# Router logits of 15 token tiles: from TensorE (turns and 8-column matmuls) to VectorE (multiply-and-sum) in a fused attention, MLP and expert kernel

## The chip, the cores and the metric

One core of a Trainium2 chip runs the whole kernel as one program. The metric is the device time of one execution in microseconds (us); lower is better.

## The reference, cut to what matters

Three layers follow each other: a sparse attention, a gated MLP on the normed rows, and a top-1 mixture of experts whose router reads the MLP's output rows. What the change touches is the line with `logits`.

```python
x = attention(q, k, v)                                  # 2304 tokens x 512
x = silu(rmsnorm(x) @ w_gate) * (rmsnorm(x) @ w_val) @ w_out   # inner width 1536
logits = x @ router_w + router_bias[modality_id]        # router_w: 512 x 8
e_idx = argmax(logits, axis=1)
gate_w = softmax(logits)[row, e_idx]
out[row] = gate_w * (relu(x @ w1[e_idx]) @ w2[e_idx])
```

All products are in fp32 precision: a large operand is split into a high and a low part (`_hi`, `_lo`) and three matmuls take the place of one.

## The kernel before, in words

**Chunks, tiles and steps.** The MLP takes the 2304 tokens in NC = 6 chunks (0 to 5) of 384 tokens; a chunk is TT = 3 tiles of 128 tokens. In each chunk it goes over the inner width in FT = 12 steps f of 128 columns. The order of the work is written out by hand, for each engine in its own queue, by a clock of half steps: a step has 6 of them (`at(c, f, sub, half)`), a chunk 72. Engines don't share a clock; the numbers only set the order of instructions in each queue, and semaphores do the rest. In one step TensorE (PE) makes the gate product (12 matmuls, half steps 0 and 1, L1100), the value product (12 matmuls, half steps 2 and 3, L1100) and the down product of the step before (9 matmuls, half steps 4 and 5, L1139); the last step of a chunk has two down products.

**The loop between engines.** ScalarE takes tanh of the gate product (L1276). VectorE multiplies it into the gate (`scale_gate`, L1418, half step 2), forms h with the value product (`form_h`, L1424, half step 4), ScalarE rounds h to its high part (L1280), and VectorE takes the low part (`h_split`, L1429, half step 5). PE's gate product of step f + 1 waits for `scale_gate` of f, its value product of f + 1 for `form_h` of f, and the down product of f for `h_split` of f. GpSimd (POOL) splits each block of `w_out` into `out_hi` (L936) and `out_lo` (L938) once a step. SyncE (SP) issues the loads and the stores of the y tiles to the scratch rows x2.

**Other work.** The attention of later batches is spread over the steps of chunks 0 to 3. At each chunk's end VectorE finds the norms of the next chunk (`roots` L1384 to L1395, `normalise_x` L1405, `x_split` L1412); POOL squares its rows (L918 to L925).

**The router's logits before.** The y of chunk c (ys, 3 tiles) is evacuated by ScalarE at the start of chunk c + 1 (L1288). During chunk c + 1 each of its tiles is turned by PE with 4 transposes (`turn_y`, L1150), evacuated by ScalarE (L1293), multiplied by the router's weights in 4 matmuls of 8 columns (`logits`, L1159; each leaves two records), and VectorE adds the bias (`add_bias`, L1437). So 15 tiles (those of chunks 0 to 4) pass through PE; the 3 tiles of chunk 5 are done after the MLP, and stay as they are. These turns and products share PSUM bank 7 with the attention and the norms.

**What follows.** In step 3 of chunk 5 (HOT_1, its half step 23 counted from 0) VectorE starts the early routing on the 15 tiles (`one_hot`, L595 to L605); PE counts it (L652, L653) at the start of the value product of step 4. The experts' loop follows the MLP.

Of the kernel before, what the change touches and what calls it, by code (L numbers as in the profile page):

```python
# [13 lines left out]
KT = DM // P  # L14
# [9 lines left out]
G = B * NG  # L24
SM = 4
# [30 lines left out]
def at(c, f, sub, half=0):  # L56
    return EARLY + SPAN * c + 6 * f + 2 * sub + half
# [29 lines left out]
def qk_ticks(b, hp):  # L87
# [3 lines left out]
    if s < EARLY:  # L91
# [20 lines left out]

SS = {0: 16, **{c + 1: at(c, 9, 2) for c in range(NC - 1)}}
SPREAD = {c: s + (2 if c == 0 else 6) for c, s in SS.items()}
Y_TILE = {(c, t): at(c + 1, 3 + 2 * t, 2) if c < NC - 2 else at(c + 1, 1 + t, 0)
          for c in range(NC - 1) for t in range(TT)}
LOGITS = {k: s + 2 for k, s in Y_TILE.items()}
SS_AT = by_tick((c, s) for c, s in SS.items())
SPREAD_AT = by_tick((c, s) for c, s in SPREAD.items())
Y_AT = by_tick((k, s) for k, s in Y_TILE.items())  # L120
LOGITS_AT = by_tick((k, s) for k, s in LOGITS.items())
BANK7 = [x for s in range(TICKS) for x in
         [("p", j) for j in TURN_AT.get(s, [])] + [("o", j) for j in PV_AT.get(s, []) if s >= EARLY]
         + [("ss", c) for c in SS_AT.get(s, []) if c] + [("rb", c) for c in SPREAD_AT.get(s, []) if c]
         + [("y", k) for k in Y_AT.get(s, [])] + [("lg", k) for k in LOGITS_AT.get(s, [])]]
# [27 lines left out]
def fused_kernel(nc, q, k, v, w_gate, w_val, w_out, rms_g, modality_id, router_w, router_bias, w1, w2, x2, out):  # L153
# [4 lines left out]
    with ctx:  # L158
# [61 lines left out]
        hh = [res.put(f"h_hi{i}", [P, CH], f32r) for i in range(2)]  # L220
        hl = [alias(f"h_lo{i}", hf_at + i * CH * 4, [P, CH], f32r) for i in range(2)]
        yT_at = res.at
        yT = res.put("yT", [P, KT, P])
        sq_at = res.at
        sq = res.put("sq", [P, CH])
        diag = alias("diagonals", sq_at, [P, TT, P])
# [15 lines left out]
        vstr = [res.put(f"vstr{i}", [SQ, 2, SU * D]) for i in range(2)]  # L242
        qT = [res.put(f"qT{i}", [P, S]) for i in range(2)]
        kT = [res.put(f"kT{i}", [P, WIN + S]) for i in range(2)]
        sm = [res.put(f"sm{i}", [P, 512]) for i in range(SM - 1)] + [alias("sm_early", yT_at, [P, 512])]
        pt = [res.put(f"pt{i}", [P, 4 * LQ]) for i in range(2)]
        mask_loc = res.put("mask_loc", [LQ, 2, P])
        mask_str = res.put("mask_str", [SQ, SQ])
# [160 lines left out]
        s_ye = sem("y_evacuated")  # L409
        s_x2 = sem("y_stored")  # L410
        s_bu = sem("bias_built")
        s_yt = sem("y_tile_turned")
        s_yte = sem("yT_evacuated")
        s_lg = sem("logits_of_tile")
        s_le = sem("logits_read")

        SQS = 2 * KT - 2
# [332 lines left out]
        def front_sp(sp):  # L750
# [91 lines left out]
            for s in range(TICKS):  # L842
                for b, hp in QK_LOAD_AT.get(s, []):
                    qk_loads(b, hp)
                for b, hp in V_LOAD_AT.get(s, []):
                    v_loads(b, hp)
                if s >= EARLY:
                    c, f, sub, half = step_of(s)
                    if (sub, half) == (0, 0) and FT * c + f + 1 < FT * NC:
                        out_load(FT * c + f + 1)  # L850
                    if c and (f, sub, half) == (0, 2, 0):
                        store(c - 1)
                if s == W_LOAD_1:
                    early_weights(sp)
            store(NC - 1)
# [107 lines left out]
        def front_pe(pe):  # L963

            def bank_7_free(what):

                before = BEFORE7[what]
                if before is None:
                    return
                if before[0] == "p":  # L970
                    pe.wait_ge(s_pe, before[1] + 1)
                elif before[0] == "o":
                    pe.wait_ge(s_oe, before[1] + 1)
                elif before[0] == "ss":
                    pe.wait_ge(s_nv, before[1] + 1)
                elif before[0] == "rb":
                    pe.wait_ge(s_xn, KT * before[1] + KT)
                elif before[0] == "y":
                    pe.wait_ge(s_yte, TT * before[1][0] + before[1][1] + 1)
                else:  # L980
                    pe.wait_ge(s_le, TT * before[1][0] + before[1][1] + 1)

            def residues():
                pe.wait_ge(s_ms, 2)
# [156 lines left out]
                if ts[-1] == TT - 1:  # L1141
                    mm.then_inc(s_y, 1)

            def turn_y(c, t):

                if t == 0:
                    pe.wait_ge(s_ye, c + 1)
                bank_7_free(("y", (c, t)))
                for kk in range(KT):
                    mm = pe.transpose(ps[:, 7, kk * P:(kk + 1) * P], ys[:, t, kk * P:(kk + 1) * P], ident[:, :])  # L1150
                mm.then_inc(s_yt, 1)

            def logits(c, t):
                bank_7_free(("lg", (c, t)))
                if c == 0 and t == 0:
                    pe.wait_ge(s_small, 48)
                pe.wait_ge(s_yte, TT * c + t + 1)
                for kk in range(KT):
# [15 lines left out]
            for s in range(TICKS):  # L1174
                if s < EARLY:
                    for key in QK_AT.get(s, []):
                        turn_qk(*key)
                for j in SCORE_AT.get(s, []):
                    score(j)
                for j in TURN_AT.get(s, []):  # L1180
                    turn_probs(j)
                for j in PV_AT.get(s, []):
                    values(j)
                if s >= EARLY:
                    for key in QK_AT.get(s, []):
# [7 lines left out]
                for key in Y_AT.get(s, []):
                    turn_y(*key)
                for key in LOGITS_AT.get(s, []):
                    logits(*key)
# [33 lines left out]
        def front_act(act):  # L1230
# [51 lines left out]
            def evac_y(c):  # L1282

                act.wait_ge(s_y, FT * c + FT)
                if c:
                    act.wait_ge(s_x2, 16 * TT * c)
                    act.wait_ge(s_yt, TT * c)
                act.activation(ys[:, :, :], ps[:, 2:2 + TT, :], ACT.Copy).then_inc(s_ye, 1)  # L1288

            def evac_yT(c, t):  # L1290

                act.wait_ge(s_yt, TT * c + t + 1)
                act.activation(yT[:, :, :].rearrange("p k n -> p (k n)"), ps[:, 7, :],  # L1293
                               ACT.Copy).then_inc(s_yte, 1)

            for s in range(TICKS):
                c, f, sub, half = step_of(s) if s >= EARLY else (0, 0, -1, 0)
# [8 lines left out]
                if s >= EARLY:  # L1306
                    for key in QK_AT.get(s, []):
                        dst, src = evac_qk(act, *key)
                        act.activation(dst, src, ACT.Copy).then_inc(s_qe, 1)
                for key in Y_AT.get(s, []):  # L1310
                    evac_yT(*key)
                if s == SPREAD[0] + 1:
                    x_split(0)
                for j in EXPS_AT.get(s, []):
# [13 lines left out]
        def front_dve(dve):  # L1328
# [100 lines left out]
                dve.tensor_tensor(hl[n % 2][:, :], hf[n % 2][:, :], hh[n % 2][:, :].bitcast(f32),  # L1429
                                  ALU.subtract).then_inc(s_hl, 1)  # L1430

            def add_bias(c, t):
                i = TT * c + t
                if i == 0:
                    dve.wait_ge(s_bu, 6)
                dve.wait_ge(s_lg, i + 1)
                dve.tensor_tensor(logit[:, i, :], ps[:, 7, 0:E], bias_t[:, i, :], ALU.add).then_inc(s_le, 1)  # L1437

            for s in range(TICKS):
                c, f, sub, half = step_of(s) if s >= EARLY else (0, 0, -1, 0)  # L1440
# [485 lines left out]
```

## Time and profile before

| | us |
|---|---|
| median of 3 runs | 930.52 (927.36 to 930.64) |
| the profiled execution, its time | 929.51 |
| its span | 927.7 |
| PE busy | 898.6 (97%) |
| DVE busy | 456.4 (49%) |
| ACT busy | 360.9 (39%) |
| POOL busy | 308.1 (33%) |

A row of instructions gives line, engine, operation, the tile written and the tiles read, their shapes and the count; behind the bar it has the busy time in us, the mean of one in ns and the idle time of the engine before them. A row of the timeline gives start, duration, and, in square brackets, the idle time before it with what released it. PEld is the load of TensorE's weights; PEclk is the granted clock of TensorE as a share of full speed.

### The profile page before, as it was taken

How to read it: one execution, taken by the hardware profiler on the slowest of the kernel's cores; microseconds unless marked ns; L12 is line 12 of the kernel's file. 1: busy time of each engine (PE TensorE's matmuls, PEld its weight loads, DVE VectorE, ACT ScalarE, POOL GpSimd, SP SyncE). 2: the span in 40 equal slices, each digit the busy share in tenths (PEclk: the TensorE clock that was granted, in tenths of full speed). 3: DMA queues.
4: the chain of work that ended last, by engine and by line, in shares of the span. 5: the costliest groups of instructions: out<-in, count | busy, mean ns of one | idle time of the engine just before them, and what ended most of it. 6: DMA issues, size and time to landing. Idle time of an engine off the chain costs nothing.

```text
span 927.7 us, 15901 instructions
## 1 busy us (share of the span) xinstructions
PE 898.6 (97%) x5433; PEld 767.6 (83%) x5433; DVE 456.4 (49%) x1239; ACT 360.9 (39%) x935; POOL 308.1 (33%) x366
## 2 busy tenths in 40 slices
PE   8989999999999999999999999999789999999996
PEld 5657898888878888799999999998678888888884
DVE  5864555433454345522433343774754466446651
ACT  5866413544444444421121131242243355335430
POOL 2734762344233342344234233240502222212221
PEclk9999999999999999999999999999889999999998
DMA  8972212222113211211121121610836355515521
GB/s 180 276 188 77 58 51 65 66 65 73 49 44 107 61 27 32 67 36 36 35 80 35 39 75 35 222 51 35 302 135 242 129 182 189 201 48 197 194 74 35
DMA packets 74486, 94.95 MB, mean 102 GB/s; under 512 B 38701, under 2 KB 42797, under 8 KB 74416
## 3 DMA queue, kind: packets, MB, share of 16 engines
q1 hardware_dynamic: 70656, 82.51, 29.2%
q0 software_dynamic: 3760, 11.54, 3.6%
q8 instruction: 40, 0.66, 0.3%
q14 instruction: 30, 0.25, 0.1%
HBM read 84.59 MB, written 10.22 MB: 102 GB/s over the span
## 4 chain that ended last, share of the span: by engine, by line
PE 90%; DVE 4%; ACT 1%; issue 1%; POOL 1%; DMA 1%; ACTq 0%; POOLq 0%; DVEq 0%
PE ps L1100 34%; PE ps L1139 15%; PE ps L1575 13%; PE ps L1590 11%; PE ps L1032 3%; PE ps L1061 2%; PE ps L1602 2%; PE ps L1042 2%; PE ps L1009 2%; PE ps L1166 1%; PE ps L1159 1%; PE ps L569 1%; PE ps L1150 1%; DMA xg<-x_rows,idx_gather 1%; DVE h_lo L1429 0%
## 5 line engine op out<-in xcount | busy, mean ns | idle before, releaser
L1418 DVE SCALAR_TENSOR_TENSOR h<-h,ps 128x384 f32<-128x384 f32 x72 | 39.9, 554 | 175.2 <-ACT h L1276 175.1
L906 POOL TENSOR_TENSOR sm<-sm,rinv 72x288 f32<-72x288 f32 (+1 forms) x51 | 45.6, 894 | 204.2 <-DVE rinv L1362 204.1
L1100 PE MATMUL ps<-x_hi,gate_hi 128*128 128x384 f32 x288 | 104.1, 362 | 0.0
L1100 PE MATMUL ps<-x_hi,val_hi 128*128 128x384 f32 x288 | 102.1, 354 | 0.0
L936 POOL CAST out_hi<-out_raw 128x512 fp32r<-128x512 f32 x72 | 46.6, 648 | 155.1 <-DMA out_raw<-in_moe_w_out 155.1
L1100 PE MATMUL ps<-x_hi,gate_lo 128*128 128x384 f32 x288 | 97.5, 338 | 0.0
L938 POOL TENSOR_TENSOR out_lo<-out_raw,out_hi 128x512 fp32r<-128x512 f32 x72 | 95.1, 1322 | 5.8
L1100 PE MATMUL ps<-x_hi,val_lo 128*128 128x384 f32 x288 | 96.9, 337 | 0.0
L1100 PE MATMUL ps<-x_lo,val_hi 128*128 128x384 f32 x288 | 96.9, 336 | 0.0
L1100 PE MATMUL ps<-x_lo,gate_hi 128*128 128x384 f32 x288 | 94.4, 338 | 0.0
L1139 PE MATMUL ps<-out_hi,h_hi 128*128 128x512 f32 x216 | 89.4, 414 | 2.1 <-DVE h_lo L1429 2.1
L1429 DVE TENSOR_TENSOR h_lo<-h,h_hi 128x384 fp32r<-128x384 f32 x72 | 64.4, 895 | 43.5 <-ACT h_hi L1280 43.5
L1139 PE MATMUL ps<-out_hi,h_lo 128*128 128x512 f32 x216 | 85.3, 395 | 0.0
L1139 PE MATMUL ps<-out_lo,h_hi 128*128 128x512 f32 x216 | 84.9, 393 | 0.0
L1532 POOL DMA_INDIRECT out_rows<-yo,idx_s x21 | 21.7, 1032 | 179.0 <-DVE yo L1766 177.2
L1280 ACT ACTIVATE h_hi<-h 128x384 fp32r<-128x384 f32 x72 | 37.7, 524 | 105.6 <-DVE h L1424 105.6
L1261 ACT ACTIVATE sm<-sm,nmin 72x72 f32<-72x72 f32 (+1 forms) x204 | 73.3, 363 | 12.1 <-DVE nmin L1351 12.0
L1424 DVE SCALAR_TENSOR_TENSOR h<-h,ps 128x384 f32<-128x384 f32 x72 | 39.9, 554 | 68.5 <-PE ps L1100 68.3
L1276 ACT ACTIVATE h<-ps 128x384 f32<-128x384 f32 x72 | 34.9, 484 | 98.6 <-PE ps L1100 98.4
L1739 DVE TENSOR_TENSOR w_lo<-w_raw,w_hi 128x1024 fp32r<-128x1024 f32 x60 | 69.4, 1220 | 4.2 <-ACT w_hi L1666 4.0
L1590 PE MATMUL ps<-w_hi,hT_hi 128*128 128x512 f32 x168 | 68.1, 405 | 0.0
L1590 PE MATMUL ps<-w_lo,hT_hi 128*128 128x512 f32 x168 | 66.4, 395 | 0.0
(248 smaller groups left out, 1926.2 us busy)
## 6 DMA issues: line engine op xcount, KB each, us to landing
w_raw<-in_moe_w SPq DMA_DIRECT2D x64, 512.0 KB, 6.6
out_raw<-in_moe_w_out SPq DMA_DIRECT2D x72, 256.0 KB, 2.6
x_rows<-y_tiles SPq DMA_DIRECT2D x18, 256.0 KB, 2.4
early_w_raw<-in_moe_w SPq DMA_DIRECT2D x8, 512.0 KB, 6.1
gate_raw<-in_moe_w_gate SPq DMA_DIRECT2D x4, 768.0 KB, 9.8
val_raw<-in_moe_w_val SPq DMA_DIRECT2D x4, 768.0 KB, 9.5
qk<-in_q SPq DMA_DIRECT2D x8, 288.0 KB
qk<-in_k SPq DMA_DIRECT2D x8, 288.0 KB
```

The costliest lines, as they stand in the source:

```text
L906: pool.tensor_tensor(s3, s3, rinv[0:n, i, :].unsqueeze(2).to_broadcast([n, 4, c]), ALU.mult).then_inc(s_no, 1)
L936: pool.tensor_copy(oh[i][:, :], o_raw[i][:, :]).then_inc(s_oh, 1)
L938: pool.tensor_tensor(ol[i][:, :], o_raw[i][:, :], oh[i][:, :].bitcast(f32), ALU.subtract).then_inc(s_ol, 1)
L1100: mm = pe.matmul(ps[:, bank, 0:CH], w[:, i, kk, cols], x[:, kk, :], start=(m == 0), stop=(m == n - 1))
L1139: mm = pe.matmul(ps[:, 2 + t, :], a[:, cols], w[:, :], start=(f == 0 and i == 0), stop=(f == FT - 1 and i == 2))
L1261: act.activation(s2, s2, ACT.Exp, scale=-1.0, bias=nmin[0:n, k_, i:i + 1], accum_out=rsum[0:n, k_, i:i + 1]).then_inc(s_ex, 1)
L1418: dve.scalar_tensor_tensor(out=hf[n % 2][:, :], in0=hf[n % 2][:, :], scalar=1.0, in1=ps[:, 0, 0:CH], op0=ALU.add, op1=ALU.mult).then_inc(s ...
L1424: dve.scalar_tensor_tensor(out=hf[n % 2][:, :], in0=hf[n % 2][:, :], scalar=0.5, in1=ps[:, 1, 0:CH], op0=ALU.mult, op1=ALU.mult).then_inc( ...
L1429: dve.tensor_tensor(hl[n % 2][:, :], hf[n % 2][:, :], hh[n % 2][:, :].bitcast(f32), ALU.subtract).then_inc(s_hl, 1)
L1575: mm = pe.matmul(ps[:, half, :], x[:, kk, :], w[:, kk, half * 512:(half + 1) * 512], start=(kk == 0 and n == 0), stop=(kk == KT - 1 and n ...
L1590: mm = pe.matmul(ps[:, 5, :], x[:, j, :], w[:, j, :], start=(j == 0 and n == 0), stop=(j == FJ - 1 and n == 2))
L1739: dve.tensor_tensor(lo[:, i * n:(i + 1) * n, :], raw[:, i * n:(i + 1) * n, :], hi[:, i * n:(i + 1) * n, :].bitcast(f32), ALU.subtract).the ...
```

## The change

The 15 tiles leave PE. For each tile and each of the 8 experts, VectorE multiplies the tile (128 tokens by 512) by the expert's router column, spread over all partitions, and sums along the row: 120 instructions of 512 elements, with the product written to a tile that nobody reads. The column is taken from `rw_all` [128, 512, 8] with a step of 8 elements (32 bytes). `rw_all` is loaded once, 16 KB for each of 128 partitions. Tiles 0 to 8 (chunks 0 to 2) are loaded back from the scratch rows into three buffers; tiles 9 to 14 are read where they lie. The dot products of tiles 0 to 11 stand at one per half step from step 5 of chunk 3 to step 8 of chunk 4, those of tiles 12 to 14 at three in two half steps from half step 4 to 19 of chunk 5. Each waits for the one before it. ScalarE's evacuation of y waits for the logits in chunk 5 only; PE's waits on bank 7 for turns and logits go. `sm_early` gets a place of its own in the room of `yT`.

```diff
-Y_TILE = {(c, t): at(c + 1, 3 + 2 * t, 2) if c < NC - 2 else at(c + 1, 1 + t, 0)
-          for c in range(NC - 1) for t in range(TT)}
-LOGITS = {k: s + 2 for k, s in Y_TILE.items()}
...
+RELOADED = TT * (NC - 3)
+ROUTER = at(NC - 3, 4, 0)
+DOT = {(i, e): at(NC - 3, 5, 0) + E * i + e if i < TT * (NC - 2)
+       else at(NC - 1, 0, 2) + (E * (i - TT * (NC - 2)) + e) * 2 // 3
+       for i in range(TT * (NC - 1)) for e in range(E)}
+DOT_AT = by_tick((k, s) for k, s in DOT.items())
+DOTTED_AT = by_tick((i, DOT[i, E - 1] + 1) for i in range(TT * (NC - 1)))
+RELOAD_AT = by_tick((i, DOT[i, 0] - 8) for i in range(RELOADED))
...
+                if s == ROUTER:
+                    sp.wait_ge(s_oe, G)
+                    sp.dma_start(rw_all[:, :, :].rearrange("p d e -> p (d e)"),
+                                 router_w.rearrange("d e -> (d e)").partition_broadcast(P)).then_inc(s_rwa, 16)
+                for i in RELOAD_AT.get(s, []):
+                    if i >= 3:
+                        sp.wait_ge(s_le, i - 2)
+                    sp.wait_ge(s_x2, 16 * TT * (i // TT + 1))
+                    sp.dma_start(y_again[i % 3][:, :], x2[i * P:(i + 1) * P, :]).then_inc(s_ya[i % 3], 16)
...
-            def turn_y(c, t):
...
-                    mm = pe.transpose(ps[:, 7, kk * P:(kk + 1) * P], ys[:, t, kk * P:(kk + 1) * P], ident[:, :])
...
-                    mm = pe.matmul(ps[:, 7, 0:E], yT[:, kk, :], rw[:, kk, :],
-                                   start=(kk == 0), stop=(kk == KT - 1))
...
-                    act.wait_ge(s_yt, TT * c)
+                if c > NC - 3:
+                    act.wait_ge(s_le, TT * c)
...
+            def dot(i, e):
+
+                if e == 0 and i < RELOADED:
+                    dve.wait_ge(s_ya[i % 3], 16 * (i // 3) + 16)
+                if e == 0 and i >= RELOADED:
+                    dve.wait_ge(s_ye, i // TT + 1)
+                if (i, e) == (0, 0):
+                    dve.wait_ge(s_rwa, 16)
+                if E * i + e:
+                    dve.wait_ge(s_dot, E * i + e)
+                if e == 0 and i >= 2:
+                    dve.wait_ge(s_le, i - 1)
+                y = y_again[i % 3][:, :] if i < RELOADED else ys[:, i % TT, :]
+                dve.tensor_tensor_reduce(out=unread[:, :], in0=y, in1=rw_all[:, :, e], scale=1.0, scalar=0.0,
+                                         op0=ALU.mult, op1=ALU.add,
+                                         accum_out=dots[:, i % 2, e:e + 1]).then_inc(s_dot, 1)
...
-                dve.tensor_tensor(logit[:, i, :], ps[:, 7, 0:E], bias_t[:, i, :], ALU.add).then_inc(s_le, 1)
+                dve.wait_ge(s_dot, E * i + E)
+                dve.tensor_tensor(logit[:, i, :], dots[:, i % 2, :], bias_t[:, i, :], ALU.add).then_inc(s_le, 1)
```

## Rows read from the trace of the kernel before

**Rows 1.** The page: busy time, and the chain that ended last.
```profile
PE 898.6 (97%) x5433; PEld 767.6 (83%) x5433; DVE 456.4 (49%) x1239; ACT 360.9 (39%) x935; POOL 308.1 (33%) x366
...
PE 90%; DVE 4%; ACT 1%; issue 1%; POOL 1%; DMA 1%; ACTq 0%; POOLq 0%; DVEq 0%
```
**Rows 2.** Windows: stretch, its length, busy us, PEclk, DMA share, GB/s.
```profile
415.43:524.40 108.97, 108.97 (x603) 102.15 (x603) 35.18 (x74) 21.81 (x42) 38.19 (x41) 1.00 0.16 46
...
559.32:566.90 7.58, 7.58 (x48) 7.14 (x47) 1.75 (x4) 1.62 (x3) 3.73 (x12) 1.00 0.12 35
...
580.77:587.04 6.27, 6.27 (x35) 5.88 (x34) 5.55 (x22) 0.49 (x1) 1.94 (x2) 1.00 0.45 145
```
**Rows 3.** Chain in order of time, chunks 3 to 5: start, us, what.
```profile
409.05 4.30 PE ps L1100 x24
...
524.43 4.18 PE ps L1100 x24
...
574.29 2.11 PE ps L1100 x12
```
**Rows 4.** Groups of VectorE by shape, whole span.
```profile
L1351 DVE CUSTOM_DVE_ANT_0 sm<-ps,mask_loc 96x128 f32<-96x128 f32 x92 | 21.1, 282 | 6.8 <-PE ps L1032 6.6
L1351 DVE CUSTOM_DVE_ANT_0 sm<-ps,mask_str 72x72 f32<-72x72 f32 x112 | 19.1, 224 | 9.1 <-PE ps L1032 9.1
L682 DVE TENSOR_TENSOR sel<-in_tile,star 128x120 f32<-128x120 f32 x1 | 0.4, 357 | 0.0
L690 DVE TENSOR_TENSOR sel<-hot,star 128x120 f32<-128x120 f32 x1 | 0.3, 283 | 0.0
L1793 DVE TENSOR_TENSOR before<-upto,in_tile 128x144 f32<-128x144 f32 x1 | 0.3, 309 | 0.0
L1794 DVE TENSOR_TENSOR rank<-before,ps 128x144 f32<-128x144 f32 x1 | 0.4, 416 | 0.0
```
**Rows 5.** Timeline of VectorE: two instructions linked by a semaphore.
```profile
449.88 0.16 DVE L1391 TENSOR_TENSOR newton<-newton,variance 128x3 f32<-128x3 f32 x1
450.08 0.16 DVE L1392 SCALAR_TENSOR_TENSOR root<-newton,root 128x3 f32<-128x3 f32 x1
```
**Rows 6.** Timeline of VectorE and POOL at 391 and 399 us.
```profile
391.50 0.78 DVE L1429 TENSOR_TENSOR h_lo<-h,h_hi 128x384 fp32r<-128x384 f32 x1 [0.59 <-ACT h_hi L1280]
...
399.65 1.67 DVE L1429 TENSOR_TENSOR h_lo<-h,h_hi 128x384 fp32r<-128x384 f32 x1 [0.59 <-ACT h_hi L1280]
...
391.26 0.61 POOL L936 CAST out_hi<-out_raw 128x512 fp32r<-128x512 f32 x1
...
399.62 1.29 POOL L938 TENSOR_TENSOR out_lo<-out_raw,out_hi 128x512 fp32r<-128x512 f32 x1
```
**Rows 7.** POOL by shape, 415.43 to 524.40 us.
```profile
L938 POOL TENSOR_TENSOR out_lo<-out_raw,out_hi 128x512 fp32r<-128x512 f32 x16 | 20.6, 1288 | 1.3
L936 POOL CAST out_hi<-out_raw 128x512 fp32r<-128x512 f32 x16 | 9.8, 614 | 67.4 <-DMA out_raw<-in_moe_w_out 67.4
```
**Rows 8.** Timeline of VectorE in chunk 5.
```profile
551.66 0.55 DVE L1424 SCALAR_TENSOR_TENSOR h<-h,ps 128x384 f32<-128x384 f32 x1 [1.07 <-PE ps L1100]
...
569.79 0.55 DVE L1418 SCALAR_TENSOR_TENSOR h<-h,ps 128x384 f32<-128x384 f32 x1 [3.36 <-ACT h L1276]
...
573.46 0.56 DVE L1429 TENSOR_TENSOR h_lo<-h,h_hi 128x384 fp32r<-128x384 f32 x1 [0.59 <-ACT h_hi L1280]
573.93 0.27 DVE L595 TENSOR_REDUCE top<-bias_then_logit 128x15 f32<-128x120 f32 x1
...
575.87 0.22 DVE L605 CAST hot_b<-hot 128x120 bf16<-128x120 f32 x1
```
**Rows 9.** Loads: KB each, median us to landing; and GB/s in 40 slices.
```profile
x_rows<-y_tiles SPq DMA_DIRECT2D x18, 256.0 KB, 2.4
...
GB/s 180 276 188 77 58 51 65 66 65 73 49 44 107 61 27 32 67 36 36 35 80 35 39 75 35 222 51 35 302 135 242 129 182 189 201 48 197 194 74 35
```
**Rows 10.** Window of the experts' first slots, columns as in group 2.
```profile
667.00:690.00 23.00, 19.49 (x69) 15.40 (x70) 13.26 (x14) 10.76 (x13) 4.97 (x8) 0.73 0.40 145
```

More of the change, by code:

```diff
@@ L114 @@
 SPREAD = {c: s + (2 if c == 0 else 6) for c, s in SS.items()}
-Y_TILE = {(c, t): at(c + 1, 3 + 2 * t, 2) if c < NC - 2 else at(c + 1, 1 + t, 0)
-          for c in range(NC - 1) for t in range(TT)}
-LOGITS = {k: s + 2 for k, s in Y_TILE.items()}
 SS_AT = by_tick((c, s) for c, s in SS.items())
 SPREAD_AT = by_tick((c, s) for c, s in SPREAD.items())
-Y_AT = by_tick((k, s) for k, s in Y_TILE.items())
-LOGITS_AT = by_tick((k, s) for k, s in LOGITS.items())
 BANK7 = [x for s in range(TICKS) for x in
          [("p", j) for j in TURN_AT.get(s, [])] + [("o", j) for j in PV_AT.get(s, []) if s >= EARLY]
-         + [("ss", c) for c in SS_AT.get(s, []) if c] + [("rb", c) for c in SPREAD_AT.get(s, []) if c]
-         + [("y", k) for k in Y_AT.get(s, [])] + [("lg", k) for k in LOGITS_AT.get(s, [])]]
+         + [("ss", c) for c in SS_AT.get(s, []) if c] + [("rb", c) for c in SPREAD_AT.get(s, []) if c]]
 BEFORE7 = {x: BANK7[n - 1] if n else None for n, x in enumerate(BANK7)}
@@ L222, in fused_kernel @@
         yT_at = res.at
-        yT = res.put("yT", [P, KT, P])
+        sm_early = res.put("sm_early", [P, 512])
         sq_at = res.at
@@ L244, in fused_kernel @@
         kT = [res.put(f"kT{i}", [P, WIN + S]) for i in range(2)]
-        sm = [res.put(f"sm{i}", [P, 512]) for i in range(SM - 1)] + [alias("sm_early", yT_at, [P, 512])]
+        sm = [res.put(f"sm{i}", [P, 512]) for i in range(SM - 1)] + [sm_early]
         pt = [res.put(f"pt{i}", [P, 4 * LQ]) for i in range(2)]
@@ L309, in fused_kernel @@
         at_pos_1 = alias("at_pos_1", vl_at, [P, EARLY_TILES, P], f32r)
+        ra = Region(xT_at + KT * 2 * S * 4)
+        rw_all = ra.put("router_on_all", [P, DM, E])
+        y_again = [ra.put(f"y_again{i}", [P, DM]) for i in range(3)]
+        unread = ra.put("unread", [P, DM])
+        dots = ra.put("dots", [P, 2, E])
         re = Region(xT_at)
@@ L411, in fused_kernel @@
         s_bu = sem("bias_built")
-        s_yt = sem("y_tile_turned")
-        s_yte = sem("yT_evacuated")
-        s_lg = sem("logits_of_tile")
+        s_rwa = sem("router_on_all_loaded")
+        s_ya = [sem(f"y_loaded_again{i}") for i in range(3)]
+        s_dot = sem("dot_products")
         s_le = sem("logits_read")
@@ L975, in bank_7_free @@
                     pe.wait_ge(s_nv, before[1] + 1)
-                elif before[0] == "rb":
+                else:
                     pe.wait_ge(s_xn, KT * before[1] + KT)
[L978 to L981, printed above, removed]
             def residues():
@@ L1142, in down @@
                     mm.then_inc(s_y, 1)
-            def turn_y(c, t):
[L1146 to L1149, printed above, removed]
-                    mm = pe.transpose(ps[:, 7, kk * P:(kk + 1) * P], ys[:, t, kk * P:(kk + 1) * P], ident[:, :])
[L1151 to L1158, printed above, removed]
-                    mm = pe.matmul(ps[:, 7, 0:E], yT[:, kk, :], rw[:, kk, :],
-                                   start=(kk == 0), stop=(kk == KT - 1))
-                mm.then_inc(s_lg, 1)
             def keep_busy(n):
@@ L1192, in front_pe @@
                     spread_roots(c)
[L1193 to L1196, printed above, removed]
                 if s == COUNT_1:
@@ L1286, in evac_y @@
                     act.wait_ge(s_x2, 16 * TT * c)
-                    act.wait_ge(s_yt, TT * c)
+                if c > NC - 3:
+                    act.wait_ge(s_le, TT * c)
                 act.activation(ys[:, :, :], ps[:, 2:2 + TT, :], ACT.Copy).then_inc(s_ye, 1)
[L1290 to L1294, printed above, removed]
             for s in range(TICKS):
@@ L1309, in front_act @@
                         act.activation(dst, src, ACT.Copy).then_inc(s_qe, 1)
-                for key in Y_AT.get(s, []):
-                    evac_yT(*key)
                 if s == SPREAD[0] + 1:
@@ L1430, in h_split, with add_bias @@
                                   ALU.subtract).then_inc(s_hl, 1)
-            def add_bias(c, t):
-                i = TT * c + t
+            def dot(i, e):
[13 more added lines that the diff above has]
+                                         accum_out=dots[:, i % 2, e:e + 1]).then_inc(s_dot, 1)
+            def add_bias(i):
                 if i == 0:
                     dve.wait_ge(s_bu, 6)
-                dve.wait_ge(s_lg, i + 1)
-                dve.tensor_tensor(logit[:, i, :], ps[:, 7, 0:E], bias_t[:, i, :], ALU.add).then_inc(s_le, 1)
+                dve.wait_ge(s_dot, E * i + E)
+                dve.tensor_tensor(logit[:, i, :], dots[:, i % 2, :], bias_t[:, i, :], ALU.add).then_inc(s_le, 1)
             for s in range(TICKS):
@@ L1460, in front_dve @@
                     invert(j)
-                for key in LOGITS_AT.get(s, []):
-                    add_bias(*key)
+                for key in DOT_AT.get(s, []):
+                    dot(*key)
+                for i in DOTTED_AT.get(s, []):
+                    add_bias(i)
                 for val, i in SPLIT_AT.get(s - 2, []):
```

## The prediction

> **What bounds the kernel now.** I read the page first: PE is busy 97% of the span, and 90% of the chain that ended last is PE [rows 1]. So work taken from PE is worth its full time, as long as no other engine takes its place. Then the windows of single steps: a plain step of the MLP takes 6.27 us, and a step of chunk 5 that also has one tile's turns and logits takes 7.58 [rows 2]. In order of time the chain of chunks 3 to 5 is PE throughout, product behind product [rows 3]. So the difference of 1.31 us lies on the path. VectorE is the other engine to watch: in the 16 steps that will hold most of the new work (step 5 of chunk 3 to step 8 of chunk 4, 415.43 to 524.40 us) it is busy 35.2 of 109.0 us, and POOL 38.2 [rows 2].
>
> **What is removed.** One tile costs PE 7.58 - 6.27 = 1.31 us, so 15 tiles are 19.7 us. By place: 7 tiles lie before the new work (chunk 1, chunk 2, the first one in chunk 3), 5 in the 16 steps, 3 in chunk 5. Only the first 7 are surely on the path afterwards: -9.2 us. ScalarE's 15 evacuations and VectorE's waits for the logits go too, at nothing: PE hid them.
>
> **What one dot product costs.** The same operation stands in the attention (L1351): 282 ns for 128 elements and 224 for 72 [rows 4]. That is 58 ns for 56 elements, 1.04 ns each, and 149 ns fixed; 512 contiguous elements are 0.68 us. But the router column is read with a step of 8 elements, and no row has that. The nearest rows are two pairs of small instructions of one size of which one reads an SBUF tile with a step: L682 (step 15) takes 357 ns and L690 283 for 120 elements, L1794 (step 18) 416 and L1793 309 for 144 [rows 4]. The extra is 0.62 and 0.74 ns per element. Bounds: nothing, if a step of 32 bytes on the second input is free, to 0.74 and perhaps more; I take 0.68, since both pairs agree: 0.35 us for 512. Each dot product waits for its predecessor by semaphore; linked instructions start 0.20 us apart at 0.16 each [rows 5], so 0.04 us is added. Sum: 0.68 + 0.35 + 0.04 = 1.07 us (0.72 without the step's extra).
> The Trainium skill, "Vector Engine (DVE) Microarchitecture Reference", section on measured stream behaviour (the access granule), says that a port keeps its rate only on pairs of adjacent words, gives 1.73 ns per column for one source hopping at every element, and 2.50 for steps of 24 words on both sources. By 1.73 a dot product would again be some 1.07 us, by 2.50 it would be 1.47 and the time below some 48 us longer (estimates from that page); no row here has steps in this form of instruction.
>
> **What POOL adds.** The dot product reads both inputs from SBUF, as L1429 does. L1429 takes 0.56 us alone [rows 8], but 1.67 when it starts 0.03 us after POOL's L938 (1.29 us), and it then ends 0.41 us behind it; started 0.24 us into L936 (0.61 us) it takes 0.78 [rows 6]. So VectorE waits until POOL is through, for about POOL's time less 0.15: 1.14 and 0.46, 1.6 us per step. The 9 other POOL instructions of the 16 steps are the squares: 38.2 - 20.6 - 9.8 = 7.8 us [rows 2, 7], 6.4 after the same cut. Together 16 x 1.6 + 6.4 = 32 us. About a seventh of VectorE's time is in operations with an input in PSUM that don't wait; I take 27 us (bounds: 0, if the dot product doesn't share what L1429 shares, and 32).
> The Trainium skill, "SBUF — State Buffer", who interferes with whom, has the second to issue block for the whole instruction, which would make it 1.9 us per step and some 4 us more in all (an estimate); the rows show 0.15 less per instruction.
>
> **The 16 steps.** VectorE's work: 35.2 us that it has, 7 more biases at 0.2 = 1.4, 96 dot products x 1.07 = 102.7, POOL 27: 166 us, against 109 that PE takes now and 102 without its 5 tiles. VectorE becomes the bound: some 10.4 us per step. It can't fall behind for free, since PE's gate product of the next step waits for `scale_gate`, which is queued behind the dot products, as are `form_h` and `h_split`. Start: the first dot product waits for `rw_all`. SP issues it when down(2) of chunk 3 ends, just before 409.05 less the logits, 408.3 [rows 3]. Its 2.1 MB at the highest rate of a slice, 302 GB/s, are 6.9 us, and 1.5 fixed (a 256 KB transfer takes 2.4) [rows 9]: it lands at 416.7, 1.5 us after VectorE wants it, hidden in part by the 4 us that PE leaves `scale_gate` (569.79 against the gate product at 574.29) [rows 3, 8]. 416.7 + 166.3 = 583.0. PE's gate product of step 9 needs only `scale_gate` of step 8, ahead of the last 4 dot products, `form_h`, `h_split`, a bias and some POOL: -6.6; then its value product waits 0.8 for `form_h`. PE is there at 577.2 where it was at 524.4 [rows 3]: +52.8 us. The 9 reloads of 256 KB take 2.4 us each [rows 9] and are asked for 8 half steps ahead: nothing, and SP's wait for `logits_read` ahead of them is met by then. Steps 9 to 11 hold no dot products; VectorE recovers and they stay as they are.
>
> **Chunk 5.** 24 dot products follow `form_h` of step 0 (ends at 552.2 [rows 8]) and must be done before `scale_gate` of step 3: 24 x 1.07 = 25.7, the MLP's own 5.0 (h_split, two steps of 1.67, `scale_gate`, three biases), POOL 3 x 1.6 less a seventh = 4.1. `scale_gate` ends at 587.0, and the gate product of step 4, at 574.29 now [rows 3], starts then: +12.8. The one-hot (573.93 to 576.1 [rows 8]) comes behind `h_split` of step 3, at 589.3, and ends at 591.3; PE is through the gate product at 589.2 and waits 2.1. Together +14.9.
>
> **Sum.** The profiled execution took 929.51, 1.0 less than the median and inside the runs shown: 929.5 - 9.2 + 52.8 + 14.9 = 988 us.
>
> **The rivals.**
> *The step is dear, POOL's turns cost nothing* (for: other ports than L1429's; against: same two inputs in SBUF). VectorE's 16 steps are 139.3 us instead of 166.3: +26.8 (the tail is 1 us shorter too). Chunk 5 without its 4.1: 8.7 + 2.1 = +10.8. 958 us.
> *The step is free, POOL costs* (for: no row with a step of 8 or on the second input; against: two pairs of rows). 96 x 0.72 = 69.1: sum 132.7, +20.1 with the shorter tail. Chunk 5: 24 x 0.72 = 17.3, so `scale_gate` ends at 578.6, 4.3 + 2.1 = +6.4. 947 us.
> *VectorE keeps up: faster.* One mechanism: reads at the full rate, and no waiting on POOL. Then 35.2 + 1.4 + 69.1 = 105.7 us of VectorE stand against 102.4 of PE, the 16 steps end 6.2 us earlier than now, chunk 5 is +0.2 (552.2 + 17.3 + 5.0 = 574.5) and the 2.1 at the count: 929.5 - 9.2 - 6.2 + 2.3 = 916 us. It is decided by the price of one dot product with its share of POOL: the 16 steps break even at (109.0 - 36.6) / 96 = 0.75 us; the rows say 1.07 + 0.28.
> *The step costs twice what the pairs show* (1.36 ns): a dot product of 1.42 us; 16 steps 52.8 + 96 x 0.35, less 1.4 in the tail, +85; chunk 5 14.9 + 24 x 0.35 = +23: 1029 us.
> *PE loses its clock.* With PE at work 6.3 of 10.4 us a step, its granted clock could fall, as to 0.73 in a stretch where it was busy 19.5 of 23 us with its idle time in long pieces [rows 10]. At 1.2 GHz a step is 12.5 us of PE, more than VectorE's 10.4: 16 steps +92, 1027 us. Against it: the gaps here are some 1 to 2 us each.
>
> **How the numbers follow.** Forecast (step dear, POOL in the way) 0.62; POOL free 0.10; step free 0.10; keeps up 0.07; step twice as dear 0.06; clock 0.05. 0.5% is about what a measurement of this kernel can tell from no change. Faster holds only where VectorE keeps up: 0.06, and 0.02 for a case between it and the others that lands within 0.5%; slower 0.92. The forecast's own spread is 975 to 1003 (0.62 to 0.74 per element, POOL 20 to 32 us). The range goes down to 945 (step free) and up to 1030 (twice as dear, clock); keeps up and what lies past 1030 are left out.
>
> **What the profile after would show.** Right: a dot product of about 1.03 us as shown, 1.35 to 1.4 a piece with POOL's share; steps of 10 us in chunks 3 and 4 with PE waiting for `scale_gate`, `form_h` and `h_lo`; VectorE without idle time there; POOL's L936 and L938 longer, since they wait too; the steps of chunk 2 without L1150 and L1159, 1.3 us shorter for each tile. Wrong: dot products of 0.68 us; VectorE idle in the 16 steps; a first dot product that starts long after 417 (the load of `rw_all` slow); PEclk under 1.00 in chunk 4; a wait for y tiles loaded again.

## The result, and the profile after

The changed kernel takes 987.05 us (median of 4 runs, 986.77 to 990.26) against 928.94 before (4 runs, 925.44 to 930.64): a ratio of 1.063, 95% interval 1.0594 to 1.0667. It is slower, 1 us from the forecast of 988.

The page of the changed kernel, to be held against [rows 1]: TensorE fell from 97% to 91%, VectorE rose by 149 us.

```profile
span 985.0 us, 15777 instructions
...
PE 900.8 (91%) x5253; PEld 754.4 (77%) x5253; DVE 605.5 (61%) x1479; ACT 351.5 (36%) x920; POOL 340.4 (35%) x366
```

Windows of the changed kernel; the columns are those of [rows 2]. The second is the 16 steps (from the tanh of step 5 of chunk 3 to that of step 9 of chunk 4), the third chunk 5 up to the tanh of step 5.

```profile
169.39:411.12 241.73, 237.64 (x1611) 202.81 (x1610) 104.09 (x392) 106.46 (x361) 92.19 (x100) 1.00 0.23 68
411.12:570.63 159.51, 117.30 (x544) 98.20 (x543) 154.92 (x268) 17.72 (x37) 66.02 (x43) 0.95 0.14 45
593.47:643.93 50.46, 36.22 (x160) 31.69 (x159) 43.49 (x89) 5.05 (x11) 13.45 (x19) 0.86 0.13 42
```

The same stretches of the kernel before:

```profile
166.46:417.57 251.11, 247.06 (x1695) 211.98 (x1694) 107.47 (x398) 109.80 (x368) 91.08 (x100) 1.00 0.20 56
417.57:526.58 109.01, 109.01 (x604) 102.19 (x603) 35.18 (x74) 21.82 (x43) 38.19 (x41) 1.00 0.16 46
549.50:582.92 33.42, 33.42 (x196) 31.57 (x195) 13.58 (x39) 7.08 (x15) 9.85 (x19) 1.00 0.20 63
```

The reader is to see VectorE: 35.2 of 109.0 us before, 154.9 of 159.5 after. Ahead of the dot products the kernel is 9.4 us shorter, in the 16 steps 50.5 longer, in the last stretch 17.0 longer: 58.1 in all. The spans differ by 57.3; the rest is in the loads at the start and in the experts' part, see below.

Who TensorE waited for in the changed kernel from 400 to 645 us (line, what it waited for, us in total, times, the longest):

```profile
PE ps L1117 <- DVE h L1405: 29.2, 15, 3.6
PE ps L1156 <- DVE h_lo L1416: 12.8, 10, 8.6
PE ps L1117 <- DVE h L1411: 9.0, 14, 2.2
...
PE ps L664 <- DVE hot_b L617: 2.3, 1, 2.3
```

These are `scale_gate`, `h_split` and `form_h` (L1418, L1429 and L1424 before), and the one-hot that the count waits for. The longest wait (8.6 us, over at 481.27) lies at the end of chunk 3, where VectorE also makes the norms of chunk 4. One step of VectorE and POOL shows how the time is spent (timelines, start and duration):

```profile
434.20 0.54 DVE L1405 SCALAR_TENSOR_TENSOR h<-h,ps 128x384 f32<-128x384 f32 x1
434.66 1.14 DVE L1432 CUSTOM_DVE_ANT_0 unread<-y_again,router_on_all 128x512 f32<-128x512 f32 x1
...
435.84 1.15 DVE L1432 CUSTOM_DVE_ANT_0 unread<-y_again,router_on_all 128x512 f32<-128x512 f32 x1
...
436.90 0.56 DVE L1411 SCALAR_TENSOR_TENSOR h<-h,ps 128x384 f32<-128x384 f32 x1
437.37 1.18 DVE L1432 CUSTOM_DVE_ANT_0 unread<-y_again,router_on_all 128x512 f32<-128x512 f32 x1
438.46 0.10 DVE L1432 DVE_READ_ACCUMULATOR2_ANT dots<- 128x1 f32 x1
438.46 1.27 DVE L1440 TENSOR_TENSOR bias_then_logit<-dots,bias_then_logit 128x8 f32<-128x8 f32 x1
```
```profile
436.43 1.03 POOL L957 CAST out_hi<-out_raw 128x512 fp32r<-128x512 f32 x1 [8.74 <-DMA out_raw<-in_moe_w_out]
437.55 2.16 POOL L959 TENSOR_TENSOR out_lo<-out_raw,out_hi 128x512 fp32r<-128x512 f32 x1
```

The dot products take 1.14 to 1.18 us, not 1.03. POOL's out_hi stands behind a dot product and comes through while VectorE is in L1411, which reads PSUM; its out_lo (1.29 us alone) lasts 2.16, since it stands behind the next dot product, and then it is the small bias addition, 8 elements from two SBUF tiles, that waits for it: 1.27 us where the addition from PSUM took 0.17.

### The profile page after: what moved, and what is told of

Same layout as the page of the kernel before. It is cut to its first block and busy times, and to the rows that moved or that the text cites. A ratio compares the mean times of both kernels' runs of the same rounds, so it can differ in the third digit from the quotient of the medians.

```text
span 985.0 us, 15777 instructions
## 1 busy us (share of the span) xinstructions
PE 900.8 (91%) x5253; PEld 754.4 (77%) x5253; DVE 605.5 (61%) x1479; ACT 351.5 (36%) x920; POOL 340.4 (35%) x366
## 5 line engine op out<-in xcount | busy, mean ns | idle before, releaser
L1117 PE MATMUL ps<-x_hi,gate_hi 128*128 128x384 f32 x288 | 106.8, 371 | 29.2 <-DVE h L1405 29.2
L957 POOL CAST out_hi<-out_raw 128x512 fp32r<-128x512 f32 x72 | 57.5, 798 | 183.5 <-DMA out_raw<-in_moe_w_out 183.5
L1405 DVE SCALAR_TENSOR_TENSOR h<-h,ps 128x384 f32<-128x384 f32 x72 | 39.7, 552 | 122.7 <-ACT h L1270 122.7
L959 POOL TENSOR_TENSOR out_lo<-out_raw,out_hi 128x512 fp32r<-128x512 f32 x72 | 110.8, 1538 | 5.8
L1117 PE MATMUL ps<-x_hi,val_hi 128*128 128x384 f32 x288 | 104.2, 362 | 9.0 <-DVE h L1411 9.0
L1156 PE MATMUL ps<-out_hi,h_hi 128*128 128x512 f32 x216 | 90.8, 421 | 15.0 <-DVE h_lo L1416 14.9
L1432 DVE CUSTOM_DVE_ANT_0 unread<-y_again,router_on_all 128x512 f32<-128x512 f32 x72 | 90.7, 1259 | 3.0 <-DMA router_on_all<-in_moe_w_gate 1.8
L1416 DVE TENSOR_TENSOR h_lo<-h,h_hi 128x384 fp32r<-128x384 f32 x72 | 68.7, 955 | 29.2 <-ACT h_hi L1274 29.2
L1117 PEld LDWEIGHTS ps<-x_hi,gate_hi 128*128 128x128 f32 x288 | 55.9, 194 | 39.5 <-DVE h L1405 35.6
L1117 PEld LDWEIGHTS ps<-x_hi,val_hi 128*128 128x128 f32 x288 | 54.7, 190 | 17.6 <-DVE h L1411 14.1
```

Of the source, the lines that this page charges most:

```text
L957: pool.tensor_copy(oh[i][:, :], o_raw[i][:, :]).then_inc(s_oh, 1)
L959: pool.tensor_tensor(ol[i][:, :], o_raw[i][:, :], oh[i][:, :].bitcast(f32), ALU.subtract).then_inc(s_ol, 1)
L1117: mm = pe.matmul(ps[:, bank, 0:CH], w[:, i, kk, cols], x[:, kk, :], start=(m == 0), stop=(m == n - 1))
L1156: mm = pe.matmul(ps[:, 2 + t, :], a[:, cols], w[:, :], start=(f == 0 and i == 0), stop=(f == FT - 1 and i == 2))
L1405: dve.scalar_tensor_tensor(out=hf[n % 2][:, :], in0=hf[n % 2][:, :], scalar=1.0, in1=ps[:, 0, 0:CH], op0=ALU.add, op1=ALU.mult).then_inc(s ...
L1432: dve.tensor_tensor_reduce(out=unread[:, :], in0=y, in1=rw_all[:, :, e], scale=1.0, scalar=0.0, op0=ALU.mult, op1=ALU.add, accum_out=dots[ ...
```

## The experiments

One number of a whole run can mislead here: on the chip of the experiments the kernel before ran from 921.09 to 942.32 us (23 runs beside the first four; all but one under 932). In the ten profiles the first tanh of chunk 0 starts anywhere from 61.9 us (before) to 68.3, also for kernels that are the same up to there (61.9 and 67.8 in the first two below). So each profile is also read by stretches, from the starts of the 72 tanh records (L1276 before). All in us:

| kernel | chunk 1 to step 5 of chunk 3 | 16 steps | chunk 4, 9 to 11 | chunk 5, to step 4 | to step 5 |
|---|---|---|---|---|---|
| before | 251.1 | 109.0 | 22.9 | 26.9 | 6.5 |
| changed | 241.7 | 159.5 | 22.8 | 40.9 | 9.6 |
| e1_dense | 243.5 | 121.4 | 23.0 | 30.1 | 10.5 |
| e2_nosplit | 241.8 | 142.7 | 22.3 | 38.9 | 9.5 |
| e3_dense_nosplit | 243.3 | 109.2 | 23.0 | 27.6 | 11.6 |
| e4_no_dots | 241.7 | 102.3 | 23.0 | 23.0 | 6.5 |
| e5_pe_kept | 251.0 | 161.5 | 22.9 | 41.3 | 9.6 |
| e6_mix | 252.7 | 101.3 | 22.9 | 26.9 | 6.5 |
| e8_mix7 | 249.7 | 103.3 | 23.0 | 25.6 | 6.5 |

**Contiguous columns (e1_dense).**

```diff
+                        act.activation(rw_cols[:, e, :], rw_all[:, :, e], ACT.Copy).then_inc(s_rc, 1)
...
-                dve.tensor_tensor_reduce(out=unread[:, :], in0=y, in1=rw_all[:, :, e], scale=1.0, scalar=0.0,
+                dve.tensor_tensor_reduce(out=unread[:, :], in0=y, in1=rw_cols[:, e, :], scale=1.0, scalar=0.0,
```

> The changed kernel with one thing undone: ScalarE copies each router column once into a contiguous tile (8 copies), and all 120 dot products read that. Theory (the step of 32 bytes is dear): a dot product falls from 1.08 to 1.16 us to 0.68, 120 x 0.44 = 53 us less work for VectorE, which still bounds the 16 steps through its turns with POOL; 935 to 950 us. Rival (the step is free, the instruction is simply slow with two SBUF inputs): dot products stay at 1.1 us and the time at 987.

Measured: 938.88 us (2 runs), ratio to before 1.0122 (1.0054 to 1.019). By shape, dot products of this kernel:

```profile
L1438 DVE CUSTOM_DVE_ANT_0 unread<-y_again,router_columns 128x512 f32<-128x512 f32 x72 | 61.6, 855 | 6.5 <-ACT router_columns L1310 5.0
```

The mean is 0.855 us with the waits for POOL in it; undisturbed ones take 0.68 to 0.70. The step in the router tile alone is worth 38 us in the 16 steps. The kernel is still slower than before.

**POOL out of the way (e2_nosplit).** ScalarE makes out_hi of blocks 41 to 63, POOL leaves them, and TensorE takes out_hi a second time in place of out_lo.

```diff
+                if n in BY_ACT:
+                    return
...
+                    act.activation(oh[n % NW][:, :], o_raw[n % NW][:, :], ACT.Copy).then_inc(s_oa, 1)
...
-                    for i, (a, w) in enumerate(((hh[n % 2], oh[n % NW]), (hh[n % 2], ol[n % NW]),
+                    for i, (a, w) in enumerate(((hh[n % 2], oh[n % NW]), (hh[n % 2], (oh if n in BY_ACT else ol)[n % NW]),
```

> The changed kernel, columns stepped, but in the steps with dot products (block 41 to 63 of w_out) ScalarE makes out_hi, POOL does nothing with the block, and TensorE multiplies by out_hi where it took out_lo: the low part of those blocks is left out, TensorE's work is the same. Theory (POOL and VectorE exclude each other on operations with two SBUF inputs): 23 x 1.6 us less one seventh = some 30 us less; 955 to 962 us, no dot product above 1.25 us but beside the squares. Rival (POOL isn't in the way): 987 us.

Measured: 966.61 us (2 runs), ratio 1.0421 (1.0351 to 1.0491): the theory's direction, but 5 us outside its range. The 16 steps are 16.9 us shorter (159.5 to 142.7), not 27; the squares' 6.4 us at most are still in it. Groups of VectorE by shape in the 16 steps, first of the changed kernel:

```profile
L1416 DVE TENSOR_TENSOR h_lo<-h,h_hi 128x384 fp32r<-128x384 f32 x16 | 17.6, 1101 | 0.0
...
L1440 DVE TENSOR_TENSOR bias_then_logit<-dots,bias_then_logit 128x8 f32<-128x8 f32 x11 | 6.6, 598 | 0.0
```

then of this one:

```profile
L1448 DVE CUSTOM_DVE_ANT_0 unread<-y_again,router_on_all 128x512 f32<-128x512 f32 x72 | 85.3, 1185 | 2.8 <-DMA router_on_all<-in_moe_w_gate 1.6
...
L1432 DVE TENSOR_TENSOR h_lo<-h,h_hi 128x384 fp32r<-128x384 f32 x16 | 8.9, 558 | 0.0
...
L1456 DVE TENSOR_TENSOR bias_then_logit<-dots,bias_then_logit 128x8 f32<-128x8 f32 x11 | 2.4, 219 | 0.0
```

POOL had cost h_lo 8.7 us (17.6 - 8.9) and the bias additions 4.2. The 72 dot products on reloaded tiles fell from 90.7 to 85.3 us only. With POOL gone they still take 1.18 on the mean, and 1.08 to 1.23 where no square runs beside them: that is the price of the step.

**Both (e3_dense_nosplit).** The two diffs above together.

> Both edits at once: contiguous columns, and blocks 41 to 63 of w_out split by ScalarE alone (their low part is left out). Theory: VectorE's work in the 16 steps is 36.6 + 96 x 0.72 + 6 = 112 us against 102 for TensorE, so the loss is nearly gone: 915 to 925 us, faster than before. Rival (dot products delay scale_gate, form_h and h_lo by their place in the queue even where VectorE has time): above 930 us.

Measured: 924.29 us (10 runs), ratio 0.9979 (0.9946 to 1.0012): no difference from before that can be told. The 16 steps are at 109.2, as before, not at TensorE's 102.3 (e4_no_dots). TensorE's waits in this kernel, 400 to 645 us:

```profile
PE ps L1170 <- DVE h_lo L1438: 5.3, 2, 4.9
PE ps L673 <- DVE hot_b L626: 2.7, 1, 2.7
PE ps L1128 <- DVE h L1427: 2.6, 3, 1.1
```

VectorE is busy 96.0 of the 109.2 us, and TensorE waits 6.4 of them. Most of that is one wait:

```profile
460.73 1.19 PE L1170 MATMUL ps<-out_hi,h_hi 128*128 128x512 f32 x2 [4.89 <-DVE h_lo L1438]
```

It lies at the end of chunk 3, where VectorE also makes the norms of chunk 4 and POOL's squares lengthen dot products to 1.19 us. The start, with ScalarE's copies and the router's load, costs 1.1 us. So the two costs account for the loss; what is left is mostly one place where the dot products, spread evenly, meet other work of VectorE. A spacing that spares this place was not tried with all 15 tiles.

**TensorE's part alone (e4_no_dots).** No dot products, no loads for them.

```diff
-DOT_AT = by_tick((k, s) for k, s in DOT.items())
+DOT_AT = {}
...
-                dve.tensor_tensor(logit[:, i, :], dots[:, i % 2, :], bias_t[:, i, :], ALU.add).then_inc(s_le, 1)
+                dve.tensor_scalar(logit[:, i, :], bias_t[:, i, :], 1.0, None, ALU.mult).then_inc(s_le, 1)
```

> TensorE's part of the change alone: turns and logits of the 15 tiles gone, and no dot products and no loads for them; the early routing runs on the bias alone, so the experts' part does other work and only the time up to its start is read. Theory (each tile is 1.31 us on the path everywhere, attention included): the stretch from chunk 1's first tanh to that of step 5 of chunk 5 is 15 x 1.31 = 19.7 us shorter than before, and evenly so: 9.2 before step 5 of chunk 3, 6.6 in the 16 steps, 3.9 in chunk 5. Rival (in chunks 1 to 3 the attention's waits take some back): under 8 us before step 5 of chunk 3.

Measured by stretches: 9.45 us, 6.68 and 3.97, 20.1 in all from chunk 1's first tanh (1.34 a tile). The theory holds, the rival falls: the attention takes nothing back. (The run's own 956.58 us, one run, say nothing here: with the bias alone for logits the experts' part is another.)

**VectorE's part alone (e5_pe_kept).** The kernel before with the dot products and loads of the change, TensorE keeping its turns and logits.

```diff
                 for key in LOGITS_AT.get(s, []):
                     add_bias(*key)
+                for key in DOT_AT.get(s, []):
+                    dot(*key)
+                for i in DOTTED_AT.get(s, []):
+                    take_dots(i)
```

> VectorE's part alone: the kernel before with all 120 dot products, their loads and waits added, their result not used; TensorE keeps turns and logits. Theory (VectorE bounds the 16 steps, TensorE has time there): the 16 steps stay at 159 us as in the changed kernel, only the 9.3 us before them come back: 996 us. Rival (both engines' work adds up): 987 + 19.7 = 1007 us.

Measured: 993.17 us (2 runs), ratio 1.0692 (1.0629 to 1.0756), near the theory's 996 and far from the rival's 1007. The 16 steps take 161.5 us with TensorE's tiles and 159.5 without them: of the 6.6 us taken from TensorE there, 2.0 count. In chunk 5 0.4 of 3.9 count.

**The price of a step (e7_steps).** Expert e's product reads with a step of e + 1 elements, so its logits are others.

```diff
+                st = e + 1
+                col = rw_all[:, 0:DM * st // E, :].rearrange("p d e -> p (d e)").rearrange(
+                    "p (d s) -> p d s", s=st)[:, :, 0]
+                pair = (y, col) if i % 2 == 0 else (col, y)
```

> Price list: the changed kernel, but expert e's dot product reads the router tile with a step of e + 1 elements (1 to 8) instead of always 8 with its own column, as second input in even tiles and as first in odd ones; the logits are those of other numbers. Theory (any step over one element costs the same 0.4 us and more): 0.68 us at step 1, 1.08 to 1.18 at 2 to 8, first or second input alike. Rivals: the price grows with the step; or it is there on the second input alone.

The kernel took 976.46 us (one run; with other logits its experts' part is another). Two tiles on the timeline of this kernel, with the stepped tile as second input from 484.97 us (step 1) on, and as first from 496.20 on:

```profile
484.97 0.69 DVE L1436 CUSTOM_DVE_ANT_0 unread<-y_again,router_on_all 128x512 f32<-128x512 f32 x1
...
485.70 0.69 DVE L1436 CUSTOM_DVE_ANT_0 unread<-y_again,router_on_all 128x512 f32<-128x512 f32 x1
...
486.79 0.83 DVE L1436 CUSTOM_DVE_ANT_0 unread<-y_again,router_on_all 128x512 f32<-128x512 f32 x1
...
487.67 1.07 DVE L1436 CUSTOM_DVE_ANT_0 unread<-y_again,router_on_all 128x512 f32<-128x512 f32 x1
...
489.13 1.13 DVE L1436 CUSTOM_DVE_ANT_0 unread<-y_again,router_on_all 128x512 f32<-128x512 f32 x1
...
496.20 0.69 DVE L1436 CUSTOM_DVE_ANT_0 unread<-router_on_all,y_again 128x512 f32<-128x512 f32 x1
...
496.93 0.69 DVE L1436 CUSTOM_DVE_ANT_0 unread<-router_on_all,y_again 128x512 f32<-128x512 f32 x1
...
498.01 0.84 DVE L1436 CUSTOM_DVE_ANT_0 unread<-router_on_all,y_again 128x512 f32<-128x512 f32 x1
```

The theory fell in its wording: a step of 2 costs nothing (0.69, as step 1), a step of 3 costs 0.15 us, steps of 4 to 8 cost 0.4 to 0.5 (undisturbed 1.05 to 1.20), and first or second input are alike. It is no matter of "any step", but neither does it go on growing.

**A version meant to beat both (e6_mix, e8_mix7).** VectorE takes only tiles of which it has room for, from the y tiles in place, with contiguous columns; the rest stays on TensorE. The 6-tile version:

```diff
+          for c in range(NC - 1) for t in range(TT) if c not in (2, 3)}
...
+DOT = {(i, e): at(3, 5, 0, 1) + (E * (i - 6) + e) * 5 // 3 if i < 9
+       else at(4, 0, 1, 1) + (E * (i - 9) + e) * 11 // 4
+       for i in range(6, 12) for e in range(E)}
```

> A version meant to beat both: only tiles 6 to 11 (chunks 2 and 3) go to VectorE, from where they lie, with contiguous columns, 48 dot products at 5/3 and 11/4 half steps apart; the other 9 tiles stay on TensorE; nothing is loaded back. Theory (what decides is whether VectorE's step, 1.67 + 3.6 x 0.72 + 1.6 = 5.9 us at most, stays under TensorE's 6.27): 6 x 1.31 = 7.9 us less than before, 920 to 924 us. Rival (any queue of dot products ahead of scale_gate costs): 928 us or more.

Measured: 923.52 us (12 runs), ratio 0.9959 (0.9925 to 0.9993). From chunk 1 to step 5 of chunk 5 it is 6.1 us shorter than before, of 7.9. The start of the dot products held ScalarE and VectorE for some 4 us while the router's tile was under way, but TensorE waited only 0.25 us there. The wait that counts is again at the end of chunk 3:

```profile
463.17 0.47 PE L1160 MATMUL ps<-out_hi,h_hi 128*128 128x512 f32 x1 [1.44 <-DVE h_lo L1457]
```

So the next expectation puts this wait in the wrong place. The 7-tile version starts later and adds one tile:

```diff
-DOT = {(i, e): at(3, 5, 0, 1) + (E * (i - 6) + e) * 5 // 3 if i < 9
-       else at(4, 0, 1, 1) + (E * (i - 9) + e) * 11 // 4
-       for i in range(6, 12) for e in range(E)}
+DOT = {(i, e): at(3, 5, 2) + (E * (i - 6) + e) * 3 // 2 if i < 9
+       else at(4, 0, 1, 1) + (E * (i - 9) + e) * 11 // 4 if i < 12
+       else at(5, 0, 2) + 2 * e
+       for i in DOTTED for e in range(E)}
```

> The 6-tile version with two edits: its first dot product (and ScalarE's copies of the columns) 3 half steps later, since both engines waited there for the router's load and TensorE lost 1.4 us behind h_lo, and one tile of chunk 4 (tile 14) more on VectorE, two half steps per dot product. Theory: 1.4 + 1.3 = 2.7 us below the 6-tile version's profile stretch by stretch, 918 to 922 us, ratio 0.991 to 0.995. Rival (24 dot products in 6 steps of chunk 3 are too dense beside POOL): no gain over the 6-tile version.

Measured: 923.36 us (12 runs; 916.83 to 934.6) against 929.64 of the kernel before beside it (17 runs), ratio 0.9934 (0.9902 to 0.9966). Same stretch: 408.0 us against 416.5 before, 8.4 less of 9.2, and 2.3 under the 6-tile version where 2.7 were expected. Its profile, 400 to 645 us, has one wait of TensorE left, in the same place (466.5 us):

```profile
PE ps L1162 <- DVE h_lo L1461: 0.8, 1, 0.8
```

It is faster than the kernel before by 0.7%, with the interval clear of 1, and than the changed one by far.

## Why the prediction was right

**What is removed: -9.2 us ahead of the dot products.** Right, 9.4; e4_no_dots shows it by itself.

**VectorE becomes the bound in the 16 steps: +52.8 us.** Right, 50.5. Shown from both sides: with TensorE's work put back (e5_pe_kept) the stretch grows by 2.0 of 6.6 us; with VectorE's made cheaper (e1, e2) it shrinks by 38 and 17. But terms of the sum were mis-sized and made up for each other. From the first dot product to the last bias of tile 11 VectorE took 163.5 us in the changed kernel and 145.3 in e2_nosplit, where the forecast had 166.3 of work:

- *"Sum: 0.68 + 0.35 + 0.04 = 1.07 us"* for one dot product. The fixed part and the contiguous rate were right to 0.01 (0.69, in e1 and e7). The extra for the step was 0.39 to 0.53, not 0.35. In e2 a dot product takes 1.22 us from its start to that of a next dot product, and 1.09 to that of any other instruction, which begins before the end (medians); the mean is 1.16, squares included. That is 8 us more in 96. That "both pairs agree" was partly luck: L1794 and L1793 differ in more than the step, since L1794 also reads PSUM [rows 4].
- *"I take 27 us"* for POOL in the 16 steps. Measured 17 to 18 with the squares left in, at most 25. The mechanism was right, the share that overlaps was not: "about a seventh of VectorE's time is in operations with an input in PSUM" was taken as if POOL came at random. On the timeline POOL waits for the dot product under way and gets in when that ends. For out_hi the next operation of VectorE was L1405 or L1411, with an input in PSUM, in 11 of 17 blocks (as at 436.90 us above), and then VectorE lost nothing; out_lo came before h_lo, a bias or another dot product in most steps, and those waited. POOL itself waited too: 66.0 us busy where it was 38.2.
- *"35.2 us that it has"* was some 6 us too high. In a full queue L1405 and L1411 are followed after 0.47 us by the next operation, where 35.2 holds 0.55 for each; and of `h_split` it holds 10.2 us, waits for POOL included, which the 27 counts again, where 0.47 each are 7.5. That term was not tested by a run of its own.
- VectorE stood idle for 3 us of the 163.5, where the forecast had none. The four together, 8 - 9 - 6 + 3, are the 3 us between 166.3 and 163.5.

**The load of the router's tile: a wait of 1.5 us.** Measured 1.8, on the first dot product. The timeline of the changed kernel:

```profile
410.52 1.19 DVE L1432 CUSTOM_DVE_ANT_0 unread<-y_again,router_on_all 128x512 f32<-128x512 f32 x1 [1.81 <-DMA router_on_all<-in_moe_w_gate]
```

No wait for the reloads stands in the lists of TensorE's and VectorE's waits.

**Chunk 5: +12.8 and +2.1.** Right in kind, 14.0 and 3.1. (As it was added up, 587.0 - 574.29 is 12.7.) Of the 3.1 the wait for the one-hot was 2.3; the rest is TensorE's clock, see the last section.

**The rivals.** The forecast's price for each was close: POOL free 958 (e2: 966.6), step free 947 (e1: 938.9), neither 916 (e3: 924.3). The first two miss by 8 us in opposite directions, which is again the step priced too low and POOL too high. The third misses because VectorE was late at the end of chunk 3 (4.9 us) and at the one-hot (2.7). The clock did fall (0.95 in the 16 steps, 0.86 in chunk 5, from 1.00) but cost little, 0.9 us behind the one-hot: elsewhere TensorE had the time. That rival's case, TensorE as the bound at 1027 us, did not come.

**Outside the sum.** The profile of the changed kernel reached its first tanh 4.4 us later than the one of before, made 1.5 good in chunk 0, and its experts' part was 3.7 us shorter. The first does not go with the change (the start is 61.9 in e1_dense, e5_pe_kept and e7_steps, 68.3 in e4_no_dots); between 20 and 40 us the loads ran at 170 GB/s where they had run at 241 before, which may be the cause and was not tried. The third goes with TensorE's clock in each profile: the experts' part is 344.8 us before, with 23 us of it at the lower level, 341.1 in the changed kernel and 341.2 in e2_nosplit with 17, and 338.4 in e1_dense with 5. So it belongs to the execution and not to the change, as far as one profile of each can tell. The two nearly cancel, and that the medians meet the forecast within 1 us is luck, of this kind and by the terms above; by its stretches (-9.2, +52.8, +14.9 against -9.4, +50.5, +17.0) it was good to 2 or 3 us.

## What to carry to other kernels

Work moved off the engine that bounds is worth its full time only while the engine that receives it stays under the same period; so price the step of the loop on the receiving engine first, with everything already in its queue, and move just as much as fits (here 7 of 15 tiles: 0.7% faster, all 15: 6.3% slower). Look first for the step in which the receiving engine already has extra work (here the norms at a chunk's end): in every version with dot products TensorE's longest wait in the MLP was there. Read the fp32 operands of such an instruction contiguous or with a step of 2; when a tile has to be read with a wide step many times, pay once for a contiguous copy on an idle engine (8 copies here, 120 readings). Two errors of opposite sign in a sum don't show in the total: an experiment for each term does.

## What the runs showed of the hardware

- VectorE's multiply-and-sum of 512 fp32 elements from SBUF takes 0.69 us with a step of 1 or 2 elements, 0.83 to 0.87 with 3, 1.05 to 1.20 with 4 to 8, on either input (e7_steps). The Trainium skill, "SBUF — State Buffer", section on the DMA port swizzle, speaks of lines of 16 bytes, of which two hits each are needed for the full rate; two, one to two and one fp32 element per line at steps of 2, 3 and 4 go with these times. The Trainium skill, "Vector Engine (DVE) Microarchitecture Reference", section on the access granule, asks for adjacent pairs of words; the step of 2 has none and ran at the full rate, so here the measurement differs.
- How long a stepped reading lasts goes with TensorE. In the changed kernel those with no POOL instruction beside them took 1.08 to 1.09 us where TensorE stood still for most of their time (17 of them), and 1.14 on the mean, up to 1.22, where it was at work; contiguous ones (e1_dense, e3_dense_nosplit) took 0.68 to 0.70 either way. This is read from the traces; no run was made to test it. Two neighbours, the second in a wait of TensorE:

```profile
564.68 1.14 DVE L1432 CUSTOM_DVE_ANT_0 unread<-y_tiles,router_on_all 128x512 f32<-128x512 f32 x1
...
565.86 1.08 DVE L1432 CUSTOM_DVE_ANT_0 unread<-y_tiles,router_on_all 128x512 f32<-128x512 f32 x1
...
567.47 0.45 PE L1117 MATMUL ps<-x_hi,gate_hi 128*128 128x384 f32 x1 [1.46 <-DVE h L1405]
```

- POOL and VectorE exclude each other also for the smallest operation: an addition of 8 elements from two SBUF tiles lasted 1.27 us beside out_lo, and 0.16 with POOL idle (in e3_dense_nosplit, below).

```profile
447.75 0.16 DVE L1462 TENSOR_TENSOR bias_then_logit<-dots,bias_then_logit 128x8 f32<-128x8 f32 x1
```

- TensorE's granted clock fell to the lower level for 17 us in the 16 steps, 10 of them beginning within its wait of 8.6 us, and for 14 us in chunk 5, after steps in which it had stood still several times. The product behind the one-hot's wait of 2.25 us took 3.12 us where it took 2.18 before. On the timeline of the changed kernel one sees the change from one level to the other within the product:

```profile
636.58 0.35 PE L1117 MATMUL ps<-x_lo,val_hi 128*128 128x384 f32 x1
636.77 0.42 PE L1117 MATMUL ps<-x_hi,val_lo 128*128 128x384 f32 x1
636.99 0.52 PE L1117 MATMUL ps<-x_hi,val_hi 128*128 128x384 f32 x1
```
